# Sparse attention with two gated layers: the reciprocals of the row sums are spread by one transpose and three broadcast DMAs, and each tile's work stands in another order

## The chip, the cores and the metric

One core of one Trainium2 chip runs the whole program. The metric is device time in microseconds (us) of one execution. TensorE (PE) does the matrix products, VectorE (DVE) and ScalarE (ACT) the elementwise work, GpSimd (POOL) splits operands, and the sync engine (SP) issues all DMA transfers.

## The reference

```python
# attention: q, k, v are (4, 8, 576, 64), tau = 0.02
scores = scale * np.matmul(q, k.transpose(0, 1, 3, 2))
thresh = np.max(scores, axis=-1, keepdims=True) - tau
scores = np.where(scores >= thresh, scores, -1000000000.0)
attn = np.exp(scores - np.max(scores, axis=-1, keepdims=True))
attn = attn / (np.sum(attn, axis=-1, keepdims=True) + 1e-09)
x = np.matmul(attn, v)                      # then (2304, 512)
# two layers, w_in (512, 2048), w_out (2048, 512)
x = mish(x @ w_in1) @ w_out1
h = x @ w_in2
out = (h * clip(h + 3, 0, 6) / 6) @ w_out2
```

## The kernel before

The attention works on 16 pairs of heads. The two heads of a pair have 2 x 576 rows of scores, which make nine tiles of 128 rows; the fifth (i = 4) holds the last 64 rows of one head and the first 64 of the other. I call the stretch in which the nine score tiles of pair n are made slot n (0 to 15), and its nine steps step 0 to 8. An iteration `it` of the code is two slots (`p` = 0 and 1), 18 steps; step s of an iteration is step i = s % 9 of a slot. All orders are written out by hand, one program per engine, with semaphores between them.

In a step, TensorE makes one tile of scores (four matmuls, eight in step 4, into one of three score buffers), some products with the values (`mix`), and turns (transposes) the weights of the tile two steps back (`turn`: one transpose for the last 64 columns, the tail, and four for the main columns into the single buffer `turned`). VectorE takes the maximum of the tile (L725), then weighs the tile before (`weigh`, L709: exponentials under the threshold become zero, row sums are kept), then makes the threshold. ScalarE copies the turned tail (L553), makes the exponentials of the new tile (L572), then copies the turned main part (L537). Turned tiles of a whole pair stand in `probsT`.

The products with the values of pair n are made one slot later, in slot n + 1 and the start of slot n + 2, as two halves: columns 0 to 255 (u = 0) and 256 to 575 (u = 1). Both use one bank of PSUM, `mixed`. Their keys (four blocks of 128 and one of 64) are handed to the steps by two tables:

```python
part0 = {4: (0,), 5: (1, 2), 6: (3, 4)}
part1 = {7: (0, 1), 8: (2,), 0: (3,), 1: (4,)}
```

The products are not yet divided by the row sums. VectorE forms the reciprocals of the nine tiles' sums in step 0 (128 x 9). `mixed` has the query along its free dimension, so the reciprocals must lie along a row, the same in each of 64 partitions. `spread_sums` (L389) does that on TensorE in steps 2 and 3, by four and six matmuls of the reciprocals with the identity; ScalarE copies the two results into `spread` (L565), and `scale_mixed` (L716) multiplies `mixed` by `spread` into x: u = 0 in step 6, u = 1 in step 1 of the next slot. VectorE works in order, so what stands behind a scaling waits with it.

SP loads q and k of head k of iteration `it` when POOL has finished with the buffer that they go into (`load_head` waits on `q_low_ready` and `k_low_ready` of head k - 2). POOL splits each head into a high and a low part (`split_head`: L803, L805, L807, for heads 0 and 1 L813, and L815), a slot or more ahead of its use. After the heads of iteration 0, SP issues the eight pieces of the first layer's `w_in` (L288), 4 MB, and then the heads of iteration 1.

At the attention's end the last turns and values products alternate with the first four up projections of the first layer (L462 to L464), until x is whole and the down projections start (L489). The layers are the rest of the program.

## Time and profile before

| | |
|---|---|
| median of 3 runs | 1116.96 us (1115.6 to 1117.17) |
| the profiled execution, its time and its span | 1116.74 us, 1115.0 us |
| TensorE busy | 1098.8 us, 99% of the span |
| weight loads busy | 880.3 us, 79% |
| VectorE, ScalarE, POOL busy | 423.6, 489.9, 263.5 us |
| chain that ended last | PE 97%, DVE 1%, ACT 1% |
| of it: scores L356 7%, values L409 8%, turns L368 5% and L364 3%, spreading L389 2% | |

The chain of work that ended last is followed back from the last instruction, at each step to what released it. Attention fills the first third of the span, up to about 334 us, and the layers the rest.

### The profile page before, as it was taken

To read this page: it belongs to the slowest core of one execution; us is meant where nothing else is said; L and a number is where in the kernel's file an instruction comes from. 1 tells how busy PE (TensorE), PEld (TensorE's weight loads), DVE (VectorE), ACT (ScalarE), POOL (GpSimd) and SP (SyncE) were. 2 spreads that over 40 slices of the span, in tenths; PEclk is the share of its full clock that TensorE was granted. 3 is DMA by queue.
4 is the path that set the end of the run, shared out by engine and by line. 5 is a ranking of instruction groups with operands and counts; after the bars stand their busy time and mean duration, and the time that the engine had idled before them with its cause. 6 is when DMAs were issued, how large, how long until landed. Compare 5 with 4: busy or idle time off the path is not lost.

```text
span 1115.0 us, 15233 instructions
## 1 busy us (share of the span) xinstructions
PE 1098.8 (99%) x6064; PEld 880.3 (79%) x6064; DVE 423.6 (38%) x903; ACT 489.9 (44%) x882; POOL 263.5 (24%) x179
## 2 busy tenths in 40 slices
PE   6999999999999999999999999999999999999998
PEld 5767676767668888889988888888888888888897
DVE  6878887878831211112121112123223223222222
ACT  5778787877743332223232234442233233232232
POOL 6686558556621300000000015430000000000000
PEclk9999999999999999999999999999999999999999
DMA  7432223223022000000000022300010010010010
GB/s 221 132 108 65 77 74 97 65 66 96 11 76 76 1 1 1 1 1 1 1 1 1 19 75 96 96 18 1 1 38 1 1 38 0 1 39 1 1 39 20
DMA packets 42488, 46.09 MB, mean 41 GB/s; under 512 B 3504, under 2 KB 30128, under 8 KB 42416
## 3 DMA queue, kind: packets, MB, share of 16 engines
q1 hardware_dynamic: 42416, 45.10, 13.6%
q8 instruction: 48, 0.79, 0.3%
q14 instruction: 24, 0.20, 0.1%
HBM read 40.37 MB, written 4.72 MB: 40 GB/s over the span
## 4 chain that ended last, share of the span: by engine, by line
PE 97%; DVE 1%; ACT 1%; issue 1%; DMA 0%; SPq 0%; DVEq 0%
PE banks L489 35%; PE banks L462 12%; PE banks L464 12%; PE banks L463 12%; PE banks L409 8%; PE banks L356 7%; PE banks L368 5%; PE banks L364 3%; PE banks L389 2%; DVE probs L709 0%; DVE neg_max L725 0%; ACT exps L572 0%; DMA q_raw<-qT 0%; ACT probsT L537 0%; DVE totals L741 0%
## 5 line engine op out<-in xcount | busy, mean ns | idle before, releaser
L770 DVE SCALAR_TENSOR_TENSOR g_low<-gate,g_high 128x512 fp32r<-128x512 f32 (+1 forms) x160 | 102.7, 642 | 473.2 <-ACT g_high L645 473.2
L462 PE MATMUL banks<-x_low,w_in_high 128*128 128x512 f32 (+1 forms) x640 | 235.9, 369 | 0.0
L463 PE MATMUL banks<-x_high,w_in_low 128*128 128x512 f32 (+1 forms) x640 | 235.5, 368 | 0.0
L464 PE MATMUL banks<-x_high,w_in_high 128*128 128x512 f32 (+1 forms) x640 | 235.5, 368 | 0.0
L645 ACT ACTIVATE g_high<-gate 128x512 fp32r<-128x512 f32 (+1 forms) x160 | 94.3, 589 | 309.6 <-PE banks L489 309.1
L462 PEld LDWEIGHTS banks<-x_low,w_in_high 128*128 128x128 f32 x640 | 120.6, 188 | 21.2 <-issue 0.6
L463 PEld LDWEIGHTS banks<-x_high,w_in_low 128*128 128x128 f32 x640 | 120.6, 188 | 20.5
L464 PEld LDWEIGHTS banks<-x_high,w_in_high 128*128 128x128 f32 x640 | 120.7, 189 | 20.0
L725 DVE TENSOR_REDUCE neg_max<-banks 128x1 f32<-128x576 f32 x144 | 108.7, 755 | 50.3 <-PE banks L356 50.1
L489 PE MATMUL banks<-g_low,w_out_high 128*128 128x512 f32 (+1 forms) x320 | 118.0, 369 | 0.8 <-issue 0.8
L489 PE MATMUL banks<-g_high,w_out_low 128*128 128x512 f32 (+1 forms) x320 | 117.8, 368 | 0.0
L489 PE MATMUL banks<-g_high,w_out_high 128*128 128x512 f32 (+1 forms) x320 | 117.7, 368 | 0.0
L709 DVE SCALAR_TENSOR_TENSOR probs<-banks,thresh,exps 128x576 f32<-128x576 f32 x144 | 116.3, 807 | 0.4 <-ACT exps L572 0.4
L489 PE MATMUL banks<-w_out_low,g_high 128*128 128x512 f32 x288 | 112.3, 390 | 0.0
L489 PE MATMUL banks<-w_out_high,g_low 128*128 128x512 f32 x288 | 112.3, 390 | 0.0
L489 PE MATMUL banks<-w_out_high,g_high 128*128 128x512 f32 x288 | 112.1, 389 | 0.0
L356 PE MATMUL banks<-k_high,q_stack 128*128 128x288 f32 x320 | 103.7, 341 | 7.9 <-DVE k_low L700 7.7
L572 ACT ACTIVATE exps<-banks,neg_max 128x576 f32<-128x576 f32 x144 | 106.8, 742 | 8.7 <-DVE neg_max L725 5.1
L822 POOL TENSOR_TENSOR w_in_low<-w_in_raw,w_in_high 128x1024 fp32r<-128x1024 f32 x16 | 38.2, 2385 | 292.3 <-ACT w_in_high L581 292.3
L636 ACT ACTIVATE relu<-banks,three 128x512 f32<-128x512 f32 (+1 forms) x80 | 51.9, 648 | 124.4 <-PE banks L464 124.1
L409 PE MATMUL banks<-probsT,values 128*64 128x256 f32 (+3 forms) x640 | 103.7, 425 | 0.6 <-issue 0.6
L763 DVE SCALAR_TENSOR_TENSOR gate<-relu,banks 128x512 f32<-128x512 f32 (+1 forms) x80 | 50.8, 635 | 139.1 <-ACT relu L636 139.1
(59 smaller groups left out, 1430.1 us busy)
## 6 DMA issues: line engine op xcount, KB each, us to landing
q_raw<-qT SPq DMA_DIRECT2D x64, 144.0 KB, 2.8
k_raw<-kT SPq DMA_DIRECT2D x64, 144.0 KB, 2.8
w_in_raw<-w_in SPq DMA_DIRECT2D x16, 512.0 KB, 4.3
w_out_raw<-w_out SPq DMA_DIRECT2D x16, 512.0 KB, 4.7
out<-x SPq DMA_DIRECT2D x18, 256.0 KB, 2.9
values<-v SPq DMA_DIRECT2D x16, 256.0 KB, 3.1
values<-v SPq DMA_DIRECT2D x16, 32.0 KB, 2.8
tau_in<-tau SPq DMA_DIRECT2D x1, 0.5 KB, 2.8
```

What stands on the lines that cost most here:

```text
L356: mm = nc.tensor.matmul(scores[s % 3][:, half, :], lhs, rhs[:, HALF * half:HALF * (half + 1)], start=(n == 0), stop=(n == len(products) - 1))
L368: mm = nc.tensor.transpose(turned[:, P * j:P * j + P], probs[:, s % 3, P * j:P * j + P], ident[:, :])
L409: mm = nc.tensor.matmul(mixed[u][DH * a:DH * a + DH, :], values[rows, b, j, DH * a:DH * a + DH], probsT[b][rows, a, j, PART_AT[u]:PART_AT[ ...
L462: nc.tensor.matmul(bank, w_in_high[:, t, cols], low, start=(t == 0), stop=False)
L463: nc.tensor.matmul(bank, w_in_low[:, t, cols], high, start=False, stop=False)
L464: mm = nc.tensor.matmul(bank, w_in_high[:, t, cols], high, start=False, stop=(t == KT - 1))
L489: mm = nc.tensor.matmul(dst, lhs, rhs, start=(f == 0 and n == 0), stop=(f == FT - 1 and n == 2))
L572: nc.scalar.activation(halves(exps[:, s % 2, :]), scores[s % 3], ACT.Exp, bias=neg_max[:, s % 3:s % 3 + 1], scale=1.0).then_inc(exp_ready, 1)
L645: nc.scalar.activation(g_high[:, f % 2, 0:width], gate[:, f % 2, 0:width], ACT.Copy, scale=1 / 6 if layer_of(c) else 1.0).then_inc(g_high_ ...
L709: nc.vector.scalar_tensor_tensor(out=halves(probs[:, s % 3, :]), in0=scores[s % 3], scalar=thresh[:, s % 3:s % 3 + 1], in1=halves(exps[:, ...
L725: nc.vector.tensor_reduce(neg_max[:, s % 3:s % 3 + 1], scores[s % 3], AX_XY, ALU.max, negate=True).then_inc(max_ready, 1)
L770: nc.vector.scalar_tensor_tensor(out=g_low[:, f % 2, 0:width], in0=gate[:, f % 2, 0:width], scalar=1 / 6 if layer_of(c) else 1.0, in1=f32( ...
```

## The change

Five things change. (1) `spread_sums` and its two copies go. In step 2 one transpose turns the 128 x 9 reciprocals into 9 x 128 (`turn_recips`), ScalarE copies that into `recip_rows` (`keep_recips`), and SP stores it to DRAM and loads it back, broadcast over 64 partitions, by three transfers into `spread` (`spread_recips`). (2) In a step, TensorE now turns directly behind the scores, and the values products come last. (3) ScalarE copies the turned main part ahead of the exponentials, no longer behind them. (4) On VectorE a scaling stands behind the weighing of its step, and waits for `spread_loaded` too. (5) The values keys are handed out anew, so that steps 2, 3 and 7 have none, and the attention's end is written out: the turns of the last two tiles stand together, and two up projections lie between the last reciprocals and the values products.

```diff
+            def spread_recips(pair):
+                sp.wait_ge(recip_rows_kept, pair + 1)
+                row = recip_dram[pair % 2]
+                sp.dma_start(row.rearrange("(t p) -> t p", p=P), recip_rows[:, :]).then_inc(recips_stored, 16)
+                sp.wait_ge(recips_stored, 16 * (pair + 1))
+                after(sp, x_ready, 2 * pair)
+                sp.dma_start(spread[0:DH, :], row[0:SEQ].partition_broadcast(DH)).then_inc(spread_loaded, 16)
+                sp.dma_start(spread[DH:P, 0:MAIN * P], row[SEQ + TAIL:2 * SEQ].partition_broadcast(DH)).then_inc(spread_loaded, 16)
+                sp.dma_start(spread[DH:P, MAIN * P:SEQ], row[SEQ:SEQ + TAIL].partition_broadcast(DH)).then_inc(spread_loaded, 16)
...
             for k in range(HEADS_IT):
+                if k == 3:
+                    spread_recips(0)
                 load_head(1, k)
             for it in range(2, ITS):
+                spread_recips(2 * it - 3)
                 for k in range(HEADS_IT):
+                    if k == 3:
+                        spread_recips(2 * it - 2)
                     load_head(it, k)
...
                 if g == EARLY_PIECES:
+                    spread_recips(PAIRS - 1)
                     sp.wait_ge(x_ready, 2 * PAIRS)
...
                 for half in range(2):
+                    if half == 0 and i == 3:
+                        after(pe, recip_rows_kept, t // PAIR_TILES)
...
+            def turn_recips(pair, b):
+                pe.wait_ge(recips_ready, pair + 1)
+                nc.tensor.transpose(turned_recips[recip_slot(pair)], recips[:, b, :], ident[:, :]).then_inc(recips_turned, 1)
...
-            part0 = {4: (0,), 5: (1, 2), 6: (3, 4)}
-            part1 = {7: (0, 1), 8: (2,), 0: (3,), 1: (4,)}
+            part0 = {4: (0, 1), 5: (2,), 6: (3, 4)}
+            part1 = {8: (0, 1), 0: (2,), 1: (3, 4)}
...
+                if (not first or s >= 2) and (ahead or s < 2):
+                    turn_tail(t - 2, (s - 2) % TILES_IT)
+                    if i == 2 and (not first or p == 1):
+                        turn_recips(pair, b)
+                    turn_main(t - 2, (s - 2) % TILES_IT)
...
+            up_early(0)
+            mix(ITS, last_pair - 1, 1 - last_b, 1, (2, 3, 4))
+            turn_tail(ITS * TILES_IT - 2, TILES_IT - 2)
+            turn_main(ITS * TILES_IT - 2, TILES_IT - 2)
+            turn_tail(ITS * TILES_IT - 1, TILES_IT - 1)
+            turn_main(ITS * TILES_IT - 1, TILES_IT - 1)
+            turn_recips(last_pair, last_b)
+            up_early(1)
+            up_early(2)
+            mix(ITS, last_pair, last_b, 0, range(MAIN + 1))
+            up_early(3)
+            mix(ITS, last_pair, last_b, 1, range(MAIN + 1))
...
             def scale_mixed(pair, u):
+                dve.wait_ge(spread_loaded, 48 * (pair + 1))
                 dve.wait_ge(mixed_ready, 2 * pair + u + 1)
```

TensorE before, from the second half of a step 2's scores to its turn and the next scores (the numbers behind a name tell apart buffers; 64x128 is the spreading):

```order
L356 MATMUL banks<-k_high_71,q_stack_70 128x288 [waits tail_kept]
L356 MATMUL banks<-k_low_72,q_stack_70 128x288
L389 MATMUL banks<-ident,recips 64x128 [waits x_ready,recips_ready]
L389 MATMUL banks<-ident,recips 64x128 x3
L364 MATMUL banks<-ident,probs 128x128 [waits probs_ready]
L368 MATMUL banks<-ident,probs 128x128 [waits main_kept]
L368 MATMUL banks<-ident,probs 128x128 x3
L356 MATMUL banks<-k_high_71,q_stack_70 128x288 [waits probs_ready]
```

TensorE in the changed kernel at the same place, where 9x128 is the transpose of the reciprocals:

```order
L389 MATMUL banks<-k_high_71,q_stack_70 128x288 [waits tail_kept]
L389 MATMUL banks<-k_low_72,q_stack_70 128x288
L397 MATMUL banks<-ident,probs 128x128 [waits probs_ready]
L409 MATMUL banks<-ident,recips 9x128 [waits recips_ready]
L403 MATMUL banks<-ident,probs 128x128 [waits main_kept]
L403 MATMUL banks<-ident,probs 128x128 x3
L389 MATMUL banks<-k_high_71,q_stack_70 128x288 [waits recip_rows_kept,probs_ready]
L389 MATMUL banks<-k_low_72,q_stack_70 128x288
```

The spreading has become one transpose inside the turn, and the scores of step 3 now wait until ScalarE has copied it out.

SP before, at the heads of iteration 1 (q_raw_66 takes heads 0 and 2, q_raw_67 heads 1 and 3):

```order
L267 DMA q_raw_66<-qT 64x576 [waits q_low_ready0]
L267 DMA q_raw_66<-qT 64x576
L271 DMA k_raw_68<-kT 64x576 [waits k_low_ready0]
L271 DMA k_raw_68<-kT 64x576
L267 DMA q_raw_67<-qT 64x576 [waits q_low_ready1]
L267 DMA q_raw_67<-qT 64x576
```

SP in the changed kernel, at the same place in its program:

```order
L278 DMA q_raw_66<-qT 64x576 [waits q_low_ready0]
L278 DMA q_raw_66<-qT 64x576
L282 DMA k_raw_68<-kT 64x576 [waits k_low_ready0]
L282 DMA k_raw_68<-kT 64x576
L298 DMA recip_dram<-recip_rows 9x128 [waits recip_rows_kept]
L302 DMA spread<-recip_dram 64x576 [waits recips_stored]
L303 DMA spread<-recip_dram 64x512
L304 DMA spread<-recip_dram 64x64
L278 DMA q_raw_67<-qT 64x576 [waits q_low_ready1]
```

The first store of reciprocals stands behind all transfers of head 2 of iteration 1, the last of which waits until POOL has finished head 0 of that iteration.

VectorE before, around the first half's scaling in a step 6:

```order
L725 TENSOR_REDUCE neg_max<-banks 128x1 [waits scores_ready]
L716 TENSOR_TENSOR x<-banks,spread 128x256 [waits mixed_ready]
L709 SCALAR_TENSOR_TENSOR probs,sums<-banks,thresh,exps 128x576 [waits main_turned,thresh_ready,exp_ready]
L736 TENSOR_SCALAR thresh<-neg_max,tau_abs 128x1 [waits max_ready]
L725 TENSOR_REDUCE neg_max<-banks 128x1 [waits scores_ready]
```

VectorE in the changed kernel:

```order
L761 TENSOR_REDUCE neg_max<-banks 128x1 [waits scores_ready]
L744 SCALAR_TENSOR_TENSOR probs,sums<-banks,thresh,exps 128x576 [waits main_turned,thresh_ready,exp_ready]
L752 TENSOR_TENSOR x<-banks,spread 128x256 [waits mixed_ready,spread_loaded]
L772 TENSOR_SCALAR thresh<-neg_max,tau_abs 128x1 [waits max_ready]
L761 TENSOR_REDUCE neg_max<-banks 128x1 [waits scores_ready]
```

The scaling has moved behind the weighing, and waits for the loads of `spread`.

## Rows read from the trace of the kernel before

**Rows 1.** Windows of 40 us inside the attention (busy us and instruction count per engine).

```profile
100.00:140.00 40.00, 40.00 (x305) 27.80 (x303) 32.56 (x85) 31.71 (x65) 26.75 (x22) 1.00 0.31 86
```

**Rows 2.** Timeline of TensorE over one steady slot (start, length, engine, line, operation).

```profile
200.48 0.66 PE L389 MATMUL banks<-ident,recips 128*64 128x128 f32 x8
...
201.07 0.33 PE L364 MATMUL banks<-ident,probs 128*128 128x128 f32 x1
...
202.36 0.92 PE L389 MATMUL banks<-ident,recips 128*64 128x128 f32 x12
...
211.38 1.30 PE L409 MATMUL banks<-probsT,values 128*64 128x320 f32 x8
...
218.85 0.38 PE L356 MATMUL banks<-k_high,q_stack 128*128 128x288 f32 x1
...
219.55 0.66 PE L389 MATMUL banks<-ident,recips 128*64 128x128 f32 x8
```

**Rows 3.** Timeline of slot 0, TensorE and VectorE, where no values matmul stands between.

```profile
22.93 0.38 PE L356 MATMUL banks<-k_high,q_stack 128*128 128x288 f32 x1
...
23.56 0.27 PE L364 MATMUL banks<-ident,probs 128*128 128x128 f32 x1
...
23.76 0.76 DVE L725 TENSOR_REDUCE neg_max<-banks 128x1 f32<-128x576 f32 x1 [0.29 <-PE banks L356]
...
24.43 0.81 DVE L709 SCALAR_TENSOR_TENSOR probs<-banks,thresh,exps 128x576 f32<-128x576 f32 x1
...
25.30 0.33 PE L364 MATMUL banks<-ident,probs 128*128 128x128 f32 x1
```

**Rows 4.** Timeline of ScalarE and VectorE at the attention's end.

```profile
311.74 0.82 DVE L709 SCALAR_TENSOR_TENSOR probs<-banks,thresh,exps 128x576 f32<-128x576 f32 x1 [0.39 <-ACT exps L572]
...
314.63 0.33 PE L364 MATMUL banks<-ident,probs 128*128 128x128 f32 x1
...
315.43 0.59 ACT L537 COPY probsT<-banks 128x512 f32<-128x512 f32 x1 [0.18 <-PE banks L368]
```

**Rows 5.** Timeline of SP's transfers and of POOL in slots 0 and 1.

```profile
16.45 9.06 SPq L288 DMA_DIRECT2D w_in_raw<-w_in  x8
...
42.22 1.11 SPq L271 DMA_DIRECT2D k_raw<-kT  x2
...
35.62 1.15 POOL L803 TENSOR_TENSOR q_stack<-q_raw,q_scale 128x576 fp32r<-128x576 f32 x1 [10.92 <-DMA q_raw<-qT]
...
40.78 1.41 POOL L815 TENSOR_TENSOR k_low<-k_raw,k_high 128x576 fp32r<-128x576 f32 x1
```

**Rows 6.** Times from issue to landing: the page's line, and q_raw's between 180 and 260 us.

```profile
q_raw<-qT SPq DMA_DIRECT2D x64, 144.0 KB, 2.8
...
DMA to landing us min/median/max: 2.4/2.7/3.4
```

**Rows 7.** Timeline of slot 1, VectorE's first scaling and TensorE's turn of tile 6.

```profile
38.24 0.42 DVE L716 TENSOR_TENSOR x<-banks,spread 128x256 f32<-128x256 f32 x1 [0.41 <-PE banks L409]
...
42.48 0.33 PE L364 MATMUL banks<-ident,probs 128*128 128x128 f32 x1
```

**Rows 8.** Timeline of TensorE's first scores, before its clock rises.

```profile
15.15 0.44 PE L356 MATMUL banks<-k_high,q_stack 128*128 128x288 f32 x1
15.39 0.44 PE L356 MATMUL banks<-k_low,q_stack 128*128 128x288 f32 x1
```

**Rows 9.** Timeline of POOL and SP across an odd slot.

```profile
206.00 1.42 POOL L815 TENSOR_TENSOR k_low<-k_raw,k_high 128x576 fp32r<-128x576 f32 x1 [12.15 <-ACT k_high L524]
...
221.64 1.10 SPq L271 DMA_DIRECT2D k_raw<-kT  x2
```

**Rows 10.** Timeline of TensorE from the last turns to the first down projection.

```profile
310.32 0.33 PE L364 MATMUL banks<-ident,probs 128*128 128x128 f32 x1
...
324.56 2.53 PE L409 MATMUL banks<-probsT,values 128*64 128x256 f32 x20 [0.57 <-issue]
...
333.79 0.47 PE L489 MATMUL banks<-g_low,w_out_high 128*128 128x512 f32 x1 [0.75 <-issue]
```

More of the change, by code:

```diff
@@ L142, in attention_and_layers @@
         turned = banks[:, 6, :]
+        turned_recips = [banks[0:PAIR_TILES, 2 * s, BANK - P:BANK] for s in range(3)]
         turned_tail = [banks[:, 2 * s + 1, BANK - P:BANK] for s in range(3)]
@@ L296, in _ @@
                         load_values(it - 1, k // 2)
-            for b in range(PAIRS_IT):
-                load_values(ITS - 1, b)
+            spread_recips(PAIRS - 3)
+            load_values(ITS - 1, 0)
+            spread_recips(PAIRS - 2)
+            load_values(ITS - 1, 1)
             sp.wait_ge(mixed_ready, 2 * PAIRS - 2)
@@ L398, in mix @@
                     pe.wait_ge(v_loaded[b], 32 * (it + 1 if b == 0 else it))
-                    pe.wait_ge(spread_kept, 2 * pair + 2)
+                    after(pe, x_ready, 2 * pair)
                     pe.wait_ge(main_kept, (pair + 1) * PAIR_TILES)
@@ L493, in down, with up_early @@
                     mm.then_inc(g_used, 1)
-            for s in range(PAIR_TILES + 2):
-                if s in ups_early:
-                    pe.wait_ge(tail_kept, ITS * TILES_IT - 2 + ups_early[s] // 2)
-                    up(0, ups_early[s])
-                attention_step(ITS, s, ahead=False)
-            pe.wait_ge(tail_kept, ITS * TILES_IT)
+            def up_early(f):
+                pe.wait_ge(tail_kept, ITS * TILES_IT - 2 + f // 2)
+                up(0, f)
+            last_pair, last_b = PAIRS - 1, PAIRS_IT - 1
+            up_early(0)
[10 more added lines that the diff above has]
+            mix(ITS, last_pair, last_b, 1, range(MAIN + 1))
             pe.wait_ge(main_kept, ITS * TILES_IT)
-            pe.wait_ge(x_ready, 2 * PAIRS)
+            pe.wait_ge(recip_rows_kept, PAIRS)
             for tile in range(STEPS * FT + LAG):
                 c, f = tile // FT, tile % FT
-                if tile < STEPS * FT and not (c == 0 and f in ups_early.values()):
+                if tile < STEPS * FT and not (c == 0 and f < UPS_EARLY):
                     up(c, f)
+                if tile == LAG:
+                    pe.wait_ge(x_ready, 2 * PAIRS)
                 if tile >= LAG:
@@ L553, in keep_tail, with keep_recips @@
                 nc.scalar.copy(dst, src).then_inc(tail_kept, 1)
+            def keep_recips(pair):
+                act.wait_ge(recips_turned, pair + 1)
+                after(act, recips_stored, 16 * pair)
+                nc.scalar.copy(recip_rows[:, :], turned_recips[recip_slot(pair)]).then_inc(recip_rows_kept, 1)
             rounds = {3: 2, 5: 3}
@@ L561, in attention_step @@
                 first = isinstance(it, int) and it == 0
-                if i in (2, 3) and (not first or p == 1):
-                    u, pair = i - 2, it * PAIRS_IT + p - 1
-                    act.wait_ge(spread_ready, 2 * pair + u + 1)
-                    nc.scalar.copy(spread[:, PART_AT[u]:PART_AT[u + 1]], mixed[u]).then_inc(spread_kept, 1)
                 if (not first or s >= 2) and (ahead or s < 2):
                     keep_tail(t - 2, (s - 2) % TILES_IT, it * PAIRS_IT + (s - 2) // PAIR_TILES)
+                if i == 2 and (not first or p == 1):
+                    keep_recips(it * PAIRS_IT + p - 1)
+                if (not first or s >= 2) and (ahead or s < 2):
+                    keep_main(t - 2, (s - 2) % TILES_IT)
                 if ahead:
@@ L573, in attention_step @@
                                          bias=neg_max[:, s % 3:s % 3 + 1], scale=1.0).then_inc(exp_ready, 1)
-                if (not first or s >= 2) and (ahead or s < 2):
-                    keep_main(t - 2, (s - 2) % TILES_IT)
                 if ahead and s in rounds:
@@ L727, in attention_step @@
                 pair, b = it * PAIRS_IT + p - 1, (p + 1) % 2
-                if i == 6 and (not first or p == 1):
-                    scale_mixed(pair, 0)
-                if i == 1 and not first:
-                    scale_mixed(pair - 1, 1)
                 if (not first or s >= 1) and (ahead or s < 1):
                     weigh(t - 1, (s - 1) % TILES_IT)
+                if ahead and i == 6 and (not first or p == 1):
+                    scale_mixed(pair, 0)
+                if ahead and i == 1 and not first:
+                    scale_mixed(pair - 1, 1)
                 if ahead:
@@ L742, in attention_step @@
                     dve.wait_ge(totals_ready, pair + 1)
+                    after(dve, recips_turned, pair - 1)
                     nc.vector.reciprocal(recips[:, b, :], totals[:, b, :]).then_inc(recips_ready, 1)
```

47 lines of the change are left out of this document (16 added, 31 removed).

## The prediction

> **What bounds the kernel now.** I read the windows first: inside the attention TensorE is busy for 40.00 of 40 us, VectorE for 32.56, ScalarE for 31.71 and POOL for 26.75 [rows 1]. So in the steady state each piece of TensorE's work is worth its length, until another engine's chain takes over. Then the timeline of one slot: it lasts 219.55 - 200.48 = 19.07 us, with no wait named, or 2.12 us for a tile [rows 2]. Last come the two ends of the attention and SP's queue, since the change gives SP work on which VectorE waits, and SP does its work in order [rows 5, 9].
>
> **What a slot saves.** The first spreading group holds TensorE for 201.07 - 200.48 = 0.59 us; the second is recorded at 0.92 and by the same overlap (0.66 against 0.59) holds it for 0.85 [rows 2]. Both go: 1.44 us per slot. The values groups keep their number and sizes, only their steps change. Scores behind which a turn stands directly take 23.56 - 22.93 = 0.63 us [rows 3], against 0.70 before a group of half width (219.55 - 218.85) [rows 2]; that gives 0.08 in each of steps 2, 3 and 7, which have no values now. The score group of one of these steps stood some 0.07 longer before than the rest, which I drop as well. TensorE's own work is then 19.07 - 1.44 - 0.24 - 0.07 = 17.32 us.
>
> The transpose of the reciprocals isn't in the trace. Its lower bound is a fourth of a turn's main part, below 0.1 us, its upper one the first spreading group, 0.59 us with its change of width. The copy of its result is at least as short as the tail's; the score group of step 3 waits for it. Both lie under the wait of the next paragraph; uncovered they would cost up to 0.6 us a slot.
>
> **What a slot loses.** A turn now follows the next scores directly and needs the weighing of its tile. Slot 0 shows that chain: scores end at 23.56, the maximum starts at 23.76, the weighing of the tile before at 24.43, and its turn starts at 25.30 [rows 3]. That is 1.74 us from the end of one tile's scores to the next turn. A step without values brings TensorE there in 0.63 + 0.51 (the turn) = 1.14 us, so it waits 0.6 us. This happens in step 2 (turn of tile 1 in step 3) and step 7; in step 3 the following scores are the double group, 0.5 us longer, which covers it. Exponentials come later now, behind the main copy: copy starts 0.80 behind the turn and takes 0.48 of the queue (315.43 - 314.63, and the recorded 0.59 less its overlap), exponential 0.77 to the weighing, so 2.05 us from the turn of tile t - 2 to the weighing of tile t, which is then only due 0.68 behind the maximum of t + 1 [rows 3, 4]. Only in steps 2 and 3 do the two come near each other, within 0.3 us. ScalarE is covered. A slot is thus 17.32 + 1.22 = 18.55 us, 0.52 less than before.
>
> **What happens once, in slot 1.** The broadcast of pair 0 stands in SP's program behind all four transfers of head 2 of iteration 1, and the last two of these wait for POOL's split of head 0. POOL could not begin that until 35.62, because its q came behind the 4 MB of `w_in` issued from 16.45 (10.92 us idle), and its last instruction starts at 40.78; SP issued the k pair at 42.22 for 1.11 us [rows 5]. None of this is moved by the change. So the store is issued at 43.35. A transfer lands 2.8 us after issue in the median, 2.4 to 3.4 in steady state [rows 6]; for a store of 4.6 KB and a broadcast of q_raw's very size I take 2.8. The store lands at 46.1, three broadcasts are issued 0.55 apart, the last at 47.3, and land at 50.05. Before, VectorE scaled this half at 38.24 [rows 7]; now it reaches that point at about 37, and stands for 13 us. Behind it are queued the threshold of tile 6, the maximum of tile 7 and the weighing of tile 6, for which TensorE's turn of tile 6 waits; then ScalarE starves too. From the scaling: 0.34 + 0.13 + 0.68 + 0.87 us to that turn [rows 3], so it starts at 52.07, where before it started at 42.48 [rows 7]: 9.6 us later, with the gain of slots 0 and 1 already in.
>
> TensorE stands idle for more than 12 us there. At the program's start, after 7.7 us of idling, it took 0.24 us from one 288-column matmul to the next (1.2 GHz), still at 15.15 [rows 8], where slot 0 later takes 0.63 us for four with their gaps (2.4 GHz) [rows 3]. That start lasted 9 us and had idle parts. If the lower level lasts 5 us after the stall, half of it is lost: 2.5 us, between 0 and 4.5. The Trainium skill ("TensorE: Matmul & The Clock Gate", section "What's actually happening") says that the clock falls back to 1.2 GHz after idling; no row here shows it fall.
>
> **The other slots.** In odd slots (3 to 13) the store again stands behind SP's k pair for head 2. POOL takes 221.64 - 206.00 = 15.6 us from the copy of k_high to that issue [rows 9]. In the new slot that copy ends some 4.4 us behind the turn of step 2 (1.74 to the turn of step 3, 1.28 to the exponentials, 0.64 for them, 0.68 for the copy), so the k pair goes at 4.4 + 15.6 - 18.55 = 1.5, the store at 2.6, and the broadcasts land at 2.6 + 2.8 + 1.1 + 2.8 = 9.3 us behind it; the scaling is due at 9.3. This is just in time, and I take 0. In even slots SP is free and the row lands 1.5 us early. The loads of heads that are pushed back have POOL's queue as cover, 7 us or more.
>
> **The end.** From the turn of tile 6 in slot 15 to the first down projection it was 333.79 - 310.32 = 23.47 us [rows 10]. Off come the spreading (1.44) and the idle 0.57. On come the pair of keys of step 8, which now stands behind that turn (1.30 less overlap, 1.23 [rows 2]), one key more (0.53), the last main turn, which waits for the copy of the one before (0.80 + 0.59 behind that one's turn, less the 0.68 at which it could start, and 0.06 for the release: 0.77), and the reciprocals' transpose (0.15): 24.15 us. The last broadcast queues behind four pieces of `w_out`, but two up projections, half a values product and another up projection cover it by about 1 us.
>
> **The sum.** Turn of tile 6 in slot 1: 52.07, +2.5 for the clock; 14 slots of 18.55 = 259.7; end 24.15: 338.4 against 333.79, 4.6 later. The 14 slots before held 0.9 us above 14 x 19.07 (310.32 - 42.48 = 267.84), half of which I expect again: +0.4. So +5.0 us on 1116.74, the profiled execution, which lies 0.2 below the median; as a median 1122.0.
>
> **The rivals.**
> - *The waits of steps 2 and 7 don't bind.* TensorE would get the slot down to 17.3 us: 14 x 1.22 = 17 us less, 1105. For it speaks that VectorE has 19% idle; against it the 1.74 us of rows 3. The gain of a slot has to pass 0.52 + 5.0/14 = 0.88 us before the change is not slower. Chance 0.11.
> - *The first scaling doesn't stall*, since SP or POOL gets there sooner. Then the 12.8 us from 37.2 to 50.0 and the clock's 2.5 fall away: 1107. SP's order and the landing at 35.62 speak against it. 0.07.
> - *The clock stays high*: 1119.5. 0.12.
> - *The round trip is longer.* With 3.4 us for each of the two transfers the stall grows by 1.2, and 6 odd slots lose up to 1.2 each: 1130; with 2.4, 0.8 less. From about 4.3 us each, even slots lose too. 0.14. The Trainium skill ("DMA: Bandwidth & Descriptors", section "Anatomy of one DMA") puts most of a transfer's fixed 2.0 us on the receipt of the write, and calls HBM, where this store goes, the heaviest target; by its fit both trips take 2.0 and 2.3 us, and the time is 1120.7. The trace's shortest is 2.4.
> - *As reckoned*: 0.56, own range 1118 to 1126.
>
> **Numbers.** 0.2% is about 2.2 us, what a measurement here can tell from no change: 1114.7 to 1119.2 counts as the same. Faster: the first two rivals less what falls in that band, 0.16. The same: half of the high clock and the low edges, 0.13. Slower: 0.71. The range takes in the longer trips and the near parts of the first two rivals: 1112 to 1130.
>
> **What the profile would show.** VectorE's first scaling idle for about 13 us before it, ended by a DMA of `spread`, at 50 us; 0.24 us steps of TensorE behind it; slots of 18.5 us with two waits of 0.6 on the weighing, in steps 3 and 8; no wait of the other scalings above 0.3; the first down projection near 338. Slots near 17.4, an early `spread`, or scalings that wait in every odd slot would each make me wrong.

## The result and the profile after

| | before | after |
|---|---|---|
| median, lowest and highest of 4 runs | 1116.98 us, 1115.6 to 1117.17 | 1126.98 us, 1125.66 to 1127.17 |
| span of the profiled execution | 1115.0 us | 1125.1 us |
| TensorE, VectorE, ScalarE, POOL busy | 1098.8, 423.6, 489.9, 263.5 us | 1088.5, 430.1, 483.9, 263.8 us |

The changed kernel takes 1.009 times as long (95% interval 1.0072 to 1.0107): 10.0 us more, where 5.0 were forecast (1122.0, range 1112 to 1130). So the direction was right, and one term, the slots, was off by more than the whole forecast (7.0 us).

The page of the changed kernel. In its second block each digit is a fortieth of the span, in tenths.

```profile
span 1125.1 us, 14747 instructions
...
PE 1088.5 (97%) x5760; PEld 870.5 (77%) x5760; DVE 430.1 (38%) x903; ACT 483.9 (43%) x866; POOL 263.8 (23%) x179
...
PE   6599999999999999999999999999999999999998
...
PEclk9799999999999999999999999999999999999999
...
PE 70%; DMA 1%; ACT 0%; issue 0%; SPq 0%; DVE 0%
```

TensorE does 10.3 us less work and the kernel is 10.1 us longer. The second slice (28 to 56 us) has the hole: TensorE 5, granted clock 7. The chain that ended last goes through two DMAs now; they are not in the hole but at the attention's end (below). The windows of the changed kernel show the hole (span of the window, busy us and count of each engine, granted clock, DMA share, GB/s); the third answers to [rows 1]:

```profile
40.00:52.00 12.00, 1.05 (x5) 0.93 (x5) 3.05 (x8) 1.00 (x2) 11.07 (x9) 0.61 0.40 120
52.00:60.00 8.00, 8.00 (x41) 4.40 (x39) 3.94 (x12) 5.14 (x9) 0.00 (x0) 0.73 0.00 0
100.00:140.00 40.00, 38.62 (x267) 26.91 (x266) 33.96 (x85) 31.17 (x64) 24.97 (x19) 1.00 0.32 91
```

The timeline of the changed kernel in slot 1, against [rows 5, 7]:

```profile
41.26 1.11 SPq L282 DMA_DIRECT2D k_raw<-kT  x2
42.41 0.56 SPq L298 DMA_DIRECT2D recip_dram<-recip_rows  x1
44.76 0.45 SPq L302 DMA_DIRECT2D spread<-recip_dram  x1
...
45.89 0.60 SPq L304 DMA_DIRECT2D spread<-recip_dram  x1
...
48.95 0.42 DVE L752 TENSOR_TENSOR x<-banks,spread 128x256 f32<-128x256 f32 x1 [11.85 <-DMA spread<-recip_dram]
...
50.95 0.48 PE L397 MATMUL banks<-ident,probs 128*128 128x128 f32 x1 [11.87 <-DVE probs L744]
...
54.94 0.44 PE L389 MATMUL banks<-k_low,q_stack 128*128 128x288 f32 x1
55.18 0.44 PE L389 MATMUL banks<-k_high,q_stack 128*128 128x288 f32 x1
...
60.61 0.27 PE L397 MATMUL banks<-ident,probs 128*128 128x128 f32 x1
```

The store leaves behind head 2's k pair, the row lands just before 48.95, VectorE stood for 11.85 us and TensorE for 11.87. After that TensorE runs at 1.2 GHz: 0.24 us from matmul to matmul at 55, as in [rows 8].

The end of the changed kernel, against [rows 10]:

```profile
320.10 0.33 PE L397 MATMUL banks<-ident,probs 128*128 128x128 f32 x1 [0.39 <-DVE probs L744]
...
344.02 0.47 PE L507 MATMUL banks<-g_low,w_out_high 128*128 128x512 f32 x1 [0.82 <-issue]
```

The first down projection comes at 344.02, 10.23 us later than before. Between the two rows lies the last pair's row of reciprocals (SP, VectorE and TensorE of the changed kernel):

```profile
331.24 0.30 SPq L298 DMA_DIRECT2D recip_dram<-recip_rows  x1
...
335.78 0.45 SPq L302 DMA_DIRECT2D spread<-recip_dram  x1
...
339.65 0.42 DVE L752 TENSOR_TENSOR x<-banks,spread 128x256 f32<-128x256 f32 x1 [3.33 <-DMA spread<-recip_dram]
340.13 3.06 PE L426 MATMUL banks<-probsT,values 128*64 128x320 f32 x20
```

The store stands behind four pieces of `w_out` and takes 4.54 us, and VectorE waits 3.33 us for the broadcast. TensorE's last values products start 0.50 us behind the matmul before them, where the products at 334.55 start 0.32 behind theirs: the wait reaches TensorE by some 0.2 us, and these are the DMAs of the chain. From these starts the difference adds up, and beside it stands what the prediction put in:

| stretch | before | after | difference | forecast |
|---|---|---|---|---|
| to the turn of tile 6 in slot 1 | 42.48 | 50.95 | +8.47 | +9.59 |
| lower clock behind it (60.61 - 50.95 = 9.66, against 7.18 for the same three gaps in a later slot) | 0 | 2.48 | +2.48 | +2.5 |
| 14 slots | 267.84 | 320.10 - 50.95 - 2.48 = 266.67 | -1.17 | -8.14 |
| turn of tile 6 in slot 15 to the first down projection | 23.47 | 23.92 | +0.45 | +0.68 |

Three terms hold within about 1 us. The slots don't: 7.0 us of the forecast gain are missing (the forecast had a further +0.4 for the 0.9 us that before's slots stood above their steady length). The next table shows where in a slot. Its numbers are the differences between the starts of the tail's transposes, tile after tile; 2 to 3 is from the turn in step 2 to the one in step 3.

| slot of | 7 to 8 | 8 to 0 | 0 to 1 | 1 to 2 | 2 to 3 | 3 to 4 | 4 to 5 | 5 to 6 | 6 to 7 | sum |
|---|---|---|---|---|---|---|---|---|---|---|
| before | 1.91 | 1.91 | 1.90 | 1.81 | 2.14 | 2.34 | 2.23 | 2.38 | 2.45 | 19.07 |
| after, from 89.82 | 1.74 | 2.56 | 1.97 | 2.65 | 1.75 | 1.66 | 2.29 | 1.85 | 2.43 | 18.90 |
| after, from 70.59 | 1.75 | 2.55 | 1.97 | 2.80 | 1.92 | 1.66 | 2.29 | 1.85 | 2.44 | 19.23 |

The two 0.6 us waits are there as forecast (1.74 where 1.14 is work, and 1.75 with the transpose and copy of the reciprocals in it). But a slot is 18.90, not 18.55, and six of the fourteen are 19.23. Both have a cause that can be looked for in the trace. First VectorE and POOL of the changed kernel, at the sum of totals in two neighbouring slots:

```profile
76.57 1.41 POOL L845 TENSOR_TENSOR q_stack<-q_raw,q_stack 64x576 fp32r<-64x576 f32 x1
76.62 1.39 DVE L777 TENSOR_SCALAR totals<-sums 128x9 f32<-128x9 f32 x1
...
95.86 0.16 DVE L777 TENSOR_SCALAR totals<-sums 128x9 f32<-128x9 f32 x1
```

The same instruction takes 0.16 us, or 1.39 when POOL has begun one 0.05 us before it: then it ends with POOL's (78.01 and 77.98). Behind it stand the reciprocals, the next maximum and the next weighing. The Trainium skill ("SBUF — State Buffer", section "Who interferes with whom") says that a `tensor_scalar` in VectorE's two-port mode and a GpSimd instruction lock the pair of ports they share for a whole instruction; the trace agrees in that the two end together, though it does not show in which mode the instruction runs. The run no_totals below tests it.

Second, TensorE of the changed kernel in step 5, whose values have one key of 256 columns:

```profile
123.53 0.29 PE L389 MATMUL banks<-k_low,q_stack 128*128 128x288 f32 x1
123.66 0.28 PE L397 MATMUL banks<-ident,probs 128*128 128x128 f32 x1
123.78 0.60 PE L403 MATMUL banks<-ident,probs 128*128 128x128 f32 x4
124.30 0.65 PE L426 MATMUL banks<-probsT,values 128*64 128x256 f32 x4
124.89 0.40 PE L389 MATMUL banks<-k_high,q_stack 128*128 128x288 f32 x1
125.12 0.30 PE L389 MATMUL banks<-k_low,q_stack 128*128 128x288 f32 x1
```

Values start 0.52 us behind the first main transpose, where scores start 0.35 behind it in the kernel before (here TensorE of before, step 3 to 4, and then values behind scores in step 4):

```profile
203.38 0.60 PE L368 MATMUL banks<-ident,probs 128*128 128x128 f32 x4
203.73 0.38 PE L356 MATMUL banks<-k_high,q_stack 128*128 128x288 f32 x1
...
204.74 0.29 PE L356 MATMUL banks<-k_low,q_stack 128*128 128x288 f32 x1
204.97 0.65 PE L409 MATMUL banks<-probsT,values 128*64 128x256 f32 x4
205.55 0.33 PE L364 MATMUL banks<-ident,probs 128*128 128x128 f32 x1
```

Entering the values costs 0.17 behind transposes, and 0.10 behind scores (0.23 against the 0.13 between scores). The scores that then follow values have a first gap of 0.23 instead of 0.22; against that, the tail's transpose behind scores has its main part 0.12 behind it, not 0.17. In sum +0.17 - 0.10 + 0.01 - 0.05 = +0.03 by these rounded rows; over whole steps it is 0.05 to 0.06, as the run old_table shows with equal tables. The Trainium skill ("TensorEngine Tiling (Array Packing)", section "Key Properties") says that a change of tiling mode drains TensorE; both orders have two such changes in a step with values. The trace shows no drain, only the gaps, and these depend on what stands ahead; why the gap behind transposes is the larger one is not shown.

### The profile page after: what moved, and what is told of

The parts are those of the page before. It is cut to its first block, busy times and chain, and to the rows that moved or that the text cites. A ratio compares the mean times of both kernels' runs of the same rounds, so it can differ in the third digit from the quotient of the medians.

```text
span 1125.1 us, 14747 instructions
## 1 busy us (share of the span) xinstructions
PE 1088.5 (97%) x5760; PEld 870.5 (77%) x5760; DVE 430.1 (38%) x903; ACT 483.9 (43%) x866; POOL 263.8 (23%) x179
## 4 chain that ended last, share of the span: by engine, by line
PE 70%; DMA 1%; ACT 0%; issue 0%; SPq 0%; DVE 0%
PE banks L507 35%; PE banks L480 11%; PE banks L481 11%; PE banks L482 11%; PE banks L426 1%; DMA recip_dram<-recip_rows 0%; DMA spread<-recip_dram 0%; PE banks L403 0%; ACT L684 0%; ACT probsT L568 0%; SPq L303 0%; PE banks L397 0%; ACT x L653 0%; SPq L302 0%; DVE x L752 0%
## 5 line engine op out<-in xcount | busy, mean ns | idle before, releaser
L389 PE MATMUL banks<-k_high,q_stack 128*128 128x288 f32 x320 | 106.3, 348 | 10.8 <-DVE k_low L735 7.7
```

The lines of the kernel that those rows point to most:

```text
L389: mm = nc.tensor.matmul(scores[s % 3][:, half, :], lhs, rhs[:, HALF * half:HALF * (half + 1)], start=(n == 0), stop=(n == len(products) - 1))
```

## The experiments

Each median is of 4 to 12 executions. "First down" is the start of the first down projection in its profile. The kernels from no_totals on leave out the addition of 1e-9 to the sums, except whole_sum (each sum holds the exponential of zero, so it is at least 1). In old_table one block of keys of one half of pair 14 is also added twice, 0.6 us of work.

| run | median us | ratio to before (95%) | first down | a slot |
|---|---|---|---|---|
| after | 1126.98 | 1.009 (1.0072 to 1.0107) | 344.02 | 18.90 and 19.23 |
| early_row | 1117.97 | 1.0012 (1.0002 to 1.0021) | 334.80 | 18.91 and 19.24 |
| no_totals | 1116.39 | 1.0001 (0.9992 to 1.001) | 333.50 | 18.90 |
| values_first | 1119.51 | 1.0024 (1.0015 to 1.0033) | 335.68 | 18.80 and 19.74 |
| old_table | 1109.23 | 0.9928 (0.9915 to 0.994) | 324.81 | 18.38 |
| row_first | 1111.36 | 0.9945 (0.9923 to 0.9967) | 329.23 | 18.90 |
| old_act | 1135.85 | 1.017 (1.0147 to 1.0192) | 354.48 | 20.32 |
| own_order | 1111.38 | 0.9953 (0.9938 to 0.9969) | 328.38 | 18.59 |
| even_table | 1118.57 | 1.0017 (1.0005 to 1.0029) | 335.18 | 19.12 |
| row_old_table | 1104.27 | 0.9888 (0.9875 to 0.9902) | 321.0 | 18.38 |
| whole_sum | 1108.34 | 0.9928 (0.9916 to 0.9941) | 325.1 | 18.39 and 19.21 |
| bridge_table | 1102.93 | 0.9875 (0.986 to 0.9891) | 319.7 | 18.32 |
| own_row | 1107.8 | 0.9918 (0.9905 to 0.9932) | 324.1 | 18.59 |

**The stall: early_row.**

```diff
             for k in range(HEADS_IT):
-                if k == 3:
+                if k == 2:
                     spread_recips(0)
                 load_head(1, k)
```

> The changed kernel with one move on SP: the store and the broadcasts of pair 0 stand ahead of head 2 of iteration 1, not behind it. Theory: the stall of 11.9 us in slot 1 goes, and with it the 2.4 us at the lower clock: 14.3 us less than the changed kernel's 1126.98, so 1112.7. Rival 1, the lower clock in slot 1 is not a result of the stall: only 11.9 less, 1115.1, and TensorE's matmuls still 0.24 apart somewhere in slot 1. Rival 2, POOL's late start is what holds slot 1 and shows up as a wait on q_low_ready or k_low_ready once the scaling doesn't wait: 1120 or more. The steady slots stay at 19.05 us in all of them.

Measured 1117.97, 9.0 less instead of 14.3. Timeline of SP, VectorE and TensorE in slot 1, then two windows (the granted clock is the seventh figure behind the window, 0.58 and 1.00):

```profile
31.40 0.55 SPq L298 DMA_DIRECT2D recip_dram<-recip_rows  x1
37.05 0.45 SPq L302 DMA_DIRECT2D spread<-recip_dram  x1
...
40.75 0.42 DVE L752 TENSOR_TENSOR x<-banks,spread 128x256 f32<-128x256 f32 x1 [3.56 <-DMA spread<-recip_dram]
...
42.75 0.33 PE L397 MATMUL banks<-ident,probs 128*128 128x128 f32 x1 [3.57 <-DVE probs L744]
...
43.82 2.40 PE L426 MATMUL banks<-probsT,values 128*64 128x320 f32 x8
```

```profile
43.00:47.00 4.00, 4.00 (x18) 2.10 (x17) 1.34 (x4) 2.43 (x4) 3.77 (x4) 0.58 0.30 82
47.00:60.00 13.00, 12.82 (x93) 9.04 (x91) 11.20 (x29) 10.55 (x22) 8.10 (x8) 1.00 0.34 100
```

The stall is the queue's, but its place in SP's program was not its only cause: the store still stands behind two heads and 4 MB of `w_in`, leaves at 31.40 and takes 5.65 us to land. So 3.6 us of stall are left, and with them a lower clock: eight values matmuls take 2.40 us instead of 1.30. Saved are 11.87 - 3.57 = 8.3 of stall and about 0.9 of clock. Rival 2 falls, since TensorE waits for nothing of POOL's there. Rival 1 falls with the next run, which has neither stall nor lower clock.

**The stall again: row_first** (on top of no_totals).

```diff
             for g in range(PIECES):
+                if g in (2, 4):
+                    load_head(1, g // 2 - 1)
+                if g == 4:
+                    spread_recips(0)
                 sp.dma_start(w_in_piece(w_in_raw, g), dram_in(w_in1, g)).then_inc(w_in_loaded, 16)
-            for k in range(HEADS_IT):
-                if k == 2:
-                    spread_recips(0)
+            for k in range(2, HEADS_IT):
                 load_head(1, k)
...
-            split_w_in(0, (w_in_loaded, 16 * PIECES))
             for it in range(1, ITS):
                 for s in range(TILES_IT):
                     attention_step(it, s)
+                    if it == 1 and s == 6:
+                        split_w_in(0, (w_in_loaded, 16 * PIECES))
```

The last lines are ScalarE's: it rounds the first piece of `w_in` later, since the pieces arrive later.

> no_totals, with SP's program in another order: two pieces of w_in, head 0 of iteration 1, two pieces, head 1, then the store and broadcasts of pair 0, then the last four pieces and heads 2 and 3; ScalarE rounds piece 0 of w_in in step 6 of iteration 1, not before it. Theory: in early_row the row was stored at 31.40, behind the heads and 4 MB of w_in, and took 5.65 us to land, so 3.6 us of stall were left, and 1.4 us at the lower clock behind it. Here the store goes out at about 29, the row is there at 34, before the scaling is due at 37, and both fall away: 5.0 less than no_totals, 1111.4. Rival, the row is late whatever its place, because the transfers share the engines with w_in: less than 2 us gained, with a wait on spread of over 2 us left.

Measured 1111.36, 5.03 less than no_totals. SP in row_first:

```profile
29.30 0.37 SPq L298 DMA_DIRECT2D recip_dram<-recip_rows  x1
31.20 0.45 SPq L302 DMA_DIRECT2D spread<-recip_dram  x1
```

The store now takes 1.9 us, no scaling in the slots waits for a row, the granted clock is 1.00 from 40 to 48 us, and the slot behind the turn of tile 6 is 18.92 instead of 20.50. The cause of stall and clock is settled. That 5.0 were forecast and 5.0 measured is partly luck: no_totals' executions spread over 4.2 us, and the two profiled ones differ by 4.3 (turn of tile 6 3.2 earlier, that slot 1.6 shorter, the end 0.4 longer, where TensorE waits 0.52 us for the scaling that the last row holds up). ScalarE's edit has no run of its own; in early_row TensorE's values products run through the whole of that rounding (45.05 to 46.09).

**The shared port: no_totals** (on top of early_row).

```diff
-                    nc.vector.tensor_scalar(totals[:, b, :], sums[:, b, :], 1e-9, None, ALU.add).then_inc(totals_ready, 1)
-                    dve.wait_ge(totals_ready, pair + 1)
...
-                    nc.vector.reciprocal(recips[:, b, :], totals[:, b, :]).then_inc(recips_ready, 1)
+                    nc.vector.reciprocal(recips[:, b, :], sums[:, b, :]).then_inc(recips_ready, 1)
```

> early_row, and VectorE's sum of totals (tensor_scalar over 128x9, plus 1e-9) left out, so that the reciprocals are taken of the sums themselves; the 1e-9 is left out of the computation. Theory: in every second slot that instruction takes 1.39 us instead of 0.16, because POOL holds the port they share; those slots are 19.23 us and the others 18.90. Without it all are 18.9: seven times 0.33, so 2.3 us less than early_row, 1110.4. Rival, the long record is a wait inside VectorE that TensorE doesn't feel, and the 0.33 us comes of something else that alternates, such as SP's transfers: within 0.4 us of early_row.

Measured 1116.39, 1.6 less where 2.3 were expected; the intervals of the two ratios overlap, but the slots differ plainly: behind the first, which holds the lower clock (20.50 in both runs), all thirteen are 18.9 now, where six were 19.24 and the last 18.99. The slots are 2.1 us less in sum, and the start and the end of this profile 0.8 more. The reciprocal itself, 0.21 us over the same 128x9, was never held, though seven of the sixteen lie inside an instruction of POOL.

**The same from the other side: whole_sum** puts the instruction back into row_old_table (below).

> row_old_table with the sum of totals (tensor_scalar over 128x9, plus 1e-9) put back, so nothing of the computation is left out. Theory: what it costs depends on where POOL's instructions lie when it comes: where one is running, it takes 1.3 us instead of 0.16 and the slot 0.33 more. POOL's rhythm comes from the slots, so again about every second slot or none: 1104.5 to 1106.5. Rival, the instruction itself is short and free wherever it stands, and all the gain of no_totals had another source: within 0.3 of row_old_table and no record above 0.3 us, while no_totals had gained.

Measured 1108.34, 4.1 more. Six slots are 19.21 and one 18.94 instead of 18.38, 5.6 us in all. In the profiled executions the start takes back 1.45 of them, since whole_sum's clock rose earlier (last section); whether that also makes the 4.1 of the medians is not settled. Here the instruction costs a slot 0.82, not 0.33: step 1 has one key of values, in the changed kernel two (1.96 against 2.65 us from turn to turn), so less of the delay is covered. My range was too low, since I carried over the 0.33 of another arrangement. VectorE in whole_sum, two neighbouring slots:

```profile
99.33 1.19 DVE L780 TENSOR_SCALAR totals<-sums 128x9 f32<-128x9 f32 x1
...
118.53 0.16 DVE L780 TENSOR_SCALAR totals<-sums 128x9 f32<-128x9 f32 x1
```

**The tables: old_table** (on top of no_totals), and row_old_table (on top of row_first, with the end's keys fitted).

```diff
-            part0 = {4: (0, 1), 5: (2,), 6: (3, 4)}
-            part1 = {8: (0, 1), 0: (2,), 1: (3, 4)}
+            part0 = {4: (0,), 5: (1, 2), 6: (3, 4)}
+            part1 = {7: (0, 1), 8: (2,), 0: (3,), 1: (4,)}
```

> no_totals, with the key tables of the kernel before (steps 2 and 3 without values, step 7 with two keys), the turn still ahead of the values. Theory: the wait of step 8's turn on the weighing goes (0.55 us a slot), and one more step has values, whose junctions cost some 0.06: slots of 18.4, 14 x 0.49 = 6.9 less than no_totals, 1103.5. Rival, that wait only moves, because VectorE's chain (1.75 us from scores to turn) or the scaling of step 6 comes due in step 7: less than 2 us gained.

> row_first with the key tables of the kernel before, and the end's keys fitted to them; the sum of totals (plus 1e-9) is left out here too. Theory: slots of 18.38 as in old_table and the turn of slot 1 as in row_first, with no stall: 14 x 0.52 = 7.3 less than row_first, 1104.1. Rival, without the stall the shorter slots leave POOL or SP too little time and a wait on a row or on a head comes back: 1107 or more.

Measured 1109.23 (7.2 less than no_totals) and 1104.27 (7.1 less than row_first). The wait of step 8 is gone. With the tables now equal, TensorE's two orders can be compared gap by gap, values between scores and turn (before) against values behind the turn (old_table):

| keys and columns | 1 x 320 | 1 x 320 | 1 x 320 (short) | 2 x 256 | 2 x 256 (one short) | 2 x 320 |
|---|---|---|---|---|---|---|
| before | 1.91 | 1.91 | 1.90 | 2.23 | 2.38 | 2.45 |
| old_table | 1.96 | 1.96 | 1.96 | 2.29 | 2.44 | 2.50 |

Each step with values is 0.05 to 0.06 longer when TensorE turns first. The changed kernel has six of them: 0.33 of the 0.35 us by which its slot misses 18.55. values_first, below, moves only TensorE's order back, and these steps get shorter again by as much.

**TensorE's order alone: values_first; ScalarE's alone: old_act; both: own_order** (each on top of no_totals, own_order with the old tables too; own_row is own_order with SP's program of row_first).

TensorE in values_first:

```diff
                     score_tile(it, s)
                 pair, b = it * PAIRS_IT + p - 1, (p + 1) % 2
+                if not first or p == 1:
+                    if i in part0:
+                        mix(it, pair, b, 0, part0[i])
...
                 if (not first or s >= 2) and (ahead or s < 2):
                     turn_tail(t - 2, (s - 2) % TILES_IT)
...
-                if not first or p == 1:
-                    if i in part0:
-                        mix(it, pair, b, 0, part0[i])
```

ScalarE in old_act:

```diff
-                if (not first or s >= 2) and (ahead or s < 2):
-                    keep_main(t - 2, (s - 2) % TILES_IT)
                 if ahead:
                     act.wait_ge(max_ready, t + 1)
...
+                if (not first or s >= 2) and (ahead or s < 2):
+                    keep_main(t - 2, (s - 2) % TILES_IT)
```

> no_totals, with the values products of a step between its scores and its turn, as in the kernel before; the key tables, ScalarE's order and the new path of the reciprocals stay. Theory: the turn now waits for the weighing only where neither its own step nor the one before it has values, which is step 3, so the 0.6 us of step 8 goes (0.55), and the six junctions from transposes to values and from values to scores go too (0.35): slots of 18.0, so 14 x 0.9 = 12.6 us less than no_totals, 1098. Rival 1, junctions cost nothing and the slot was mis-added: only the wait goes, 14 x 0.55 = 7.7 less, 1103. Rival 2, ScalarE's early copy now waits in front of the exponentials for the later turn, and holds the chain: slots above 18.9, no gain.

> no_totals, with ScalarE's main copy behind the exponentials again, as in the kernel before; TensorE still turns ahead of the values. Theory: ScalarE is covered in this order of TensorE, except that in the steps without values the next turn's main part waits for a copy that now comes 0.7 us later: slots 18.9 to 19.4, 1116 to 1123. Rival 1, the early copy is what delays the exponentials and makes the two 0.6 us waits: then they shrink, slots near 18.3, 1108. Rival 2, it makes no difference at all, within 1 us.

> no_totals with the whole order of the kernel before: values between scores and turn, ScalarE's main copy behind the exponentials, the old key tables (the end's keys fitted to them). What is left of the change is the transpose and the round trip through DRAM in place of the spreading. Theory: the waits of values_first came of ScalarE (its copies stood ahead of the exponentials while the turn came late in the step), so with its own order they go; of the 1.44 us of spreading, 0.4 to 0.5 are given back as the wait of step 3 on the weighing: slots of 18.1, 14 x 0.8 = 11 less than no_totals, 1105. Rival, the waits of values_first stay (the second half of the scores on the tail's copy, 0.9 us in every second slot), because the copy of the row of reciprocals stands in ScalarE's queue: slots above 18.6.

> own_order with SP's program of row_first. Theory: the 18.59 us slots of own_order stay and the 3.6 us of stall with their lower clock go: 5.0 less than own_order's 1111.4, 1106.4, so the change's order of work with the old tables (row_old_table) is 14 x 0.21 = 2.9 us better than the old order, both with the new path. Rival, the orders tie within 1 us.

Measured 1119.51, 1135.85, 1111.38 and 1107.8. The first two of my expectations failed. In the third the slot is 18.59, not 18.1, and 5.0 us were saved where 11 were expected: once a slot TensorE's main turn waits 0.4 us for ScalarE's main copy, now that no spreading stands between. The steps with values do get the 0.05 us back in values_first (1.91, 1.80 and 2.38 where no_totals has 1.97, 1.86 and 2.43), but ScalarE is late. Two waits of TensorE in values_first between 60 and 290 us (what waited, for what: us in all, times, longest):

```profile
PE banks L389 <- ACT recip_rows L591: 7.7, 12, 0.6
...
PE banks L389 <- ACT probsT L584: 5.7, 6, 0.9
```

ScalarE and TensorE at one of the six:

```profile
78.40 1.05 ACT L616 CAST w_in_high<-w_in_raw 128x1024 fp32r<-128x1024 f32 x1
...
79.78 0.40 PE L389 MATMUL banks<-k_high,q_stack 128*128 128x288 f32 x1 [0.94 <-ACT probsT L584]
```

TensorE's turn comes late in the step, so ScalarE's copies, which stand ahead of the exponentials, hold these up, and TensorE waits for the tail's copy in every second slot, the one in which ScalarE also rounds a piece of `w_in` (1.05 us, until 79.45) ahead of that copy. Rival 2 of values_first was right. In old_act it is the other way about; TensorE and ScalarE there:

```profile
105.26 0.74 ACT L607 ACTIVATE exps<-banks,neg_max 128x576 f32<-128x576 f32 x1 [0.42 <-DVE neg_max L761]
...
105.89 0.58 ACT L568 COPY probsT<-banks 128x512 f32<-128x512 f32 x1
...
106.01 0.33 PE L397 MATMUL banks<-ident,probs 128*128 128x128 f32 x1 [0.52 <-DVE probs L744]
...
106.53 0.66 PE L403 MATMUL banks<-ident,probs 128*128 128x128 f32 x4 [0.19 <-ACT probsT L568]
```

The main copy of one tile, behind the exponentials, ends at 106.47, and the next main turn waits for it, in four steps of a slot: 1.4 us. So TensorE's order and ScalarE's belong together: a new order of the one beside the old order of the other (1119.51 and 1135.85) is slower than the new orders together (1116.39). With the new path and the old tables, the two new orders have slots of 18.38 and the two old ones of 18.59 (row_old_table 1104.27, own_row 1107.8, of which the slots are the 2.9 expected). VectorE's order, part (4) of the change, is the new one in all of these runs, so what it is worth is not known.

**More even tables: even_table** (on top of no_totals) and **bridge_table** (on top of row_old_table).

even_table:

```diff
-            part1 = {8: (0, 1), 0: (2,), 1: (3, 4)}
+            part1 = {7: (0,), 8: (1,), 0: (2,), 1: (3,), 2: (4,)}
...
-                if ahead and i == 1 and not first:
+                if ahead and i == 3 and not first:
                     scale_mixed(pair - 1, 1)
```

bridge_table, whose second scaling stands in step 2 ahead of the maximum:

```diff
-            part0 = {4: (0,), 5: (1, 2), 6: (3, 4)}
+            part0 = {2: (0,), 4: (1,), 5: (2,), 6: (3, 4)}
```

> no_totals with the values' keys handed out so that only step 3 has none: two keys in step 4, one in step 5, two in step 6, then one each in steps 7, 8, 0, 1 and 2; the second scaling moves from step 1 to step 3 of VectorE. Theory: the turns of steps 3 and 8 no longer wait for the weighing (1.1 us), two more steps pay the junction of 0.055, and the scores of step 3 no longer wait 0.2 for the row's copy: slots of 17.8 to 17.9, 14 x 1.05 = 14.7 less than no_totals, 1101.7. Rival, VectorE's chain is the bound and the wait only moves to other steps: slots of 18.4 or more, 1109.

> row_old_table with the first key of the first half moved from step 4 to step 2 and one of step 5 to step 4 (step 5 has one then), and the second scaling moved on VectorE from step 1, behind the weighing, to step 2, ahead of the maximum. Theory: the values of step 2 cover the wait of step 3's turn (0.6 us) and of its scores on the row's copy (0.2): 0.55 + 0.18 less, one more junction 0.055: slots of 17.7, 14 x 0.68 = 9.5 less than row_old_table, 1094.6. Rival, the chain of one bank closes: the first half's key in step 2 waits for the second half's scaling, which waits for the values of step 1, and the maximum of step 2 waits behind that scaling: slots of 18.4 or more, no gain.

even_table measured 1118.57, 2.2 more than no_totals, with a gap of 2.89 us behind step 2. ScalarE there:

```profile
109.26 0.26 ACT L584 COPY probsT<-banks 64x128 f32<-64x128 f32 x1 [1.59 <-PE banks L426]
```

The values of step 2 still read the `probsT` into which the first tile of the next pair is copied in that same step (`keep_tail` waits for `mixed_ready`). The second half has to end in step 1. Neither my theory nor my rival had this. bridge_table respects it and measured 1102.93, 1.3 less than row_old_table and not the 9.5 expected: its slot is 18.32, which makes 0.8 us of the 1.3. The key that moved from step 5 to step 2 saves 0.43 there and costs 0.22 in step 2 (I had counted the wait on the copy of the row twice), and 0.14 comes back in steps 3 and 4.

## Why the prediction was half right

- **What happens once, in slot 1**: right in place and cause, and 1.1 us too long. Stall 11.9 against 13 us, turn of tile 6 at 50.95 against 52.07. The store left at 42.41 and not at 43.35, since the k pair ahead of it went out earlier (41.26 against 42.22), and took 2.35 us and not 2.8; the last broadcast (45.89) took about 3.0. The prediction's figures by the Trainium skill ("DMA: Bandwidth & Descriptors", section "Anatomy of one DMA"), 2.0 and 2.3 us, were measured there on transfers that GpSimd issues, and for the two trips of SP here they are 1.1 too short. early_row and row_first confirm the cause. It is luck that this term's error of 1.1 us hid part of the error of the slots.
- **The clock**: 2.5 forecast, 2.48 by the gaps; row_first has neither stall nor low clock. That the clock falls, which no row of before showed, this trace shows: granted 0.61 in the mean between 40 and 52 us, and 0.73 between 52 and 60. The length of 5 us that the prediction took for the lower level was an assumption that came out well.
- **What a slot loses, the two waits**: right. Both are in the trace, and the old tables remove one (0.52 a slot, with the gap of one more step with values in it).
- **What a slot saves**: this step failed; the slot is 18.90 and not 18.55. "The values groups keep their number and sizes, only their steps change" put their new place behind the transposes at nothing. old_table against before prices it at 0.05 to 0.06 us a step, six times, 0.33 a slot. The rest is a slip in the sum: 0.70 - 0.63 is 0.07 and not 0.08, three times. Together 14 x 0.35 = 4.9 us are missing.
- **VectorE's short instructions** were not looked at at all. This term was put at nothing. The sum of totals was 1.27 us in the kernel before, too (at 293.62, and 0.71 at 45.33), and I saw 0.9 us of odd length there without asking what it was: half of it is the slot of 293.62, where TensorE then waits 0.42 us for a scaling, the other half the slot of 45.33, where it waits for a copy of ScalarE behind the rounding of `w_in`. In the new rhythm the sum of totals meets an instruction of POOL in six steady slots: 6 x 0.33 = 2.0 us. The two together are 6.9 of the 7.0 us.
- **The other slots**: right, no scaling of an odd slot waits for its row. They do wait for TensorE's values, by up to 0.51 us, where the prediction's signs allowed 0.3. **The end**: 23.92 against 24.15, right in sum, but its cover of about 1 us for the last broadcast was not there: VectorE waits 3.33 us for it and TensorE some 0.2.
- **The rivals**: the clock staying high, the waits not binding and no stall did not happen. The longer round trip came only behind megabytes: in early_row behind `w_in` (5.65 us), and for the last pair behind `w_out` (4.54). ScalarE is covered, as I wrote, but only because its order was changed together with TensorE's (old_act, +19.5 us): the prediction gave that edit no price of its own.

The new path of the reciprocals pays once the row leaves SP early and the tables keep step 7 filled: row_old_table is 12.4 us faster than the kernel before and bridge_table 13.8, with the 1e-9 left out; whole_sum, with nothing left out, is 8.4 faster.

## What to carry to other kernels

A DMA round trip in place of engine work is priced by where its first use stands in the queues: ask what is issued ahead of it, and how many megabytes are still in flight. A group of matmuls of another shape can change its price with what stands ahead of it (here 0.17 and 0.10 us at its start), so a reordered step is to be counted gap by gap. And when a slot is now and then odd by a fraction of a microsecond, look at the shortest and longest record of each instruction: the small one that is long sometimes will be long more often in another rhythm.

## What the runs showed of the hardware

- An idle time of TensorE of only 3.57 us was followed by 1.2 GHz (early_row: granted clock 0.58 between 43 and 47 us, 1.00 again from 47). The prediction had looked for it only behind the stall of 12 us.
- A store of 4.6 KB to DRAM takes 1.2 us until the next transfer on it is issued when SP's queue is free (61.48 to 62.72 in the changed kernel), 1.9 in row_first, 2.35 behind a k pair, 4.54 behind four pieces of `w_out` (2 MB), and 5.65 behind 4 MB and two heads.
- The clock rises at a different time in executions of the same start. In row_old_table's profile TensorE's transpose at 11.71 us still has the slow record of 0.47 us, in whole_sum's the one at 11.58 has 0.33, and from there whole_sum is 1.4 us ahead. The executions of one of these two kernels differ by 0.8 and 1.9 us. TensorE in row_old_table, then in whole_sum:

```profile
11.71 0.47 PE L399 MATMUL banks<-ident,probs 128*128 128x128 f32 x1 [0.62 <-DVE probs L747]
```

```profile
11.58 0.33 PE L399 MATMUL banks<-ident,probs 128*128 128x128 f32 x1 [0.62 <-DVE probs L747]
```
